# Between the dense steps and the experts: a gather ahead of the first, held weight loads, first rows and activations by halves, fillers at y's copies

## What is computed

```python
x = attention(q, k, v)                    # 2 x 8 heads, 768 positions, 4 sinks, window 128
h = x @ w_in                              # 512 -> 2048, the dense layer
g = np.maximum(h, 0.0) + alpha * np.minimum(h, 0.0)
x = g @ w_out                             # 2048 -> 512: "y" in the kernel
logits = x @ w_gate                       # 8 experts
expert_idx = np.argmax(logits, axis=1)
for i in range(N):                        # in order of tokens
    e = expert_idx[i]
    if counts[e] < capacity:              # 384
        disp[e, counts[e]] = x[i]
        pos[i] = counts[e]; counts[e] += 1; keep[i] = True
h = np.maximum(np.einsum('ecd,edf->ecf', disp, w1), 0.0)
y = np.einsum('ecf,efd->ecd', h, w2)
out[i] = gate_w[i] * y[expert_idx[i], pos[i]]     # rows that were kept
```

## Time and profile before

| | us |
|---|---|
| median of 3 runs | 606.51 |
| lowest, highest | 605.64, 608.17 |
| the profiled execution | 607.66 |
| its span, first to last instruction | 605.9 |
| PE busy in it | 585.7 (97%) |
| mean granted clock of PE | 0.988 of full speed |

### The profile page before, as it was taken

One profiled execution on the slowest core, in us unless ns is written; L12 is line 12 of the kernel. 1 busy time (PEld: TensorE's weight loads), 2 busy tenths in 40 slices (PEclk: granted clock), 3 DMA queues, 4 the chain that ended last, 5 costly groups with the idle time before them and its releaser, 6 DMA issues.

```text
span 605.9 us, 11537 instructions
## 1 busy us (share of the span) xinstructions
PE 585.7 (97%) x3848; PEld 497.4 (82%) x3848; DVE 362.0 (60%) x1063; ACT 276.7 (46%) x681; POOL 147.2 (24%) x244
## 2 busy tenths in 40 slices
PE   8999999999999999999999999998999999989994
PEld 7787878888888888888888899987788888868883
DVE  5878886575556565766565445465826396588200
ACT  5865555342433334333432121142826487697320
POOL 5311332222111221222223100005103243453001
PEclk9999999999999999999999999989999999989998
DMA  7534443001152302010000230027836589597000
GB/s 192 151 94 151 132 126 85 1 18 38 34 158 70 89 18 71 18 36 19 36 18 2 86 123 1 2 87 227 317 136 197 189 294 371 162 393 253 18 21 19
DMA packets 73271, 67.44 MB, mean 111 GB/s; under 512 B 42884, under 2 KB 49044, under 8 KB 73200
## 3 DMA queue, kind: packets, MB, share of 16 engines
q1 hardware_dynamic: 68464, 57.50, 30.0%
q0 software_dynamic: 3680, 8.77, 4.6%
q10 hardware_dynamic: 1056, 0.26, 0.2%
HBM read 57.75 MB, written 12.06 MB: 115 GB/s over the span
## 4 chain that ended last, share of the span: by engine, by line
PE 86%; DVE 6%; issue 3%; ACT 3%; DMA 2%; POOL 0%; SPq 0%; DVEq 0%; POOLq 0%; ACTq 0%
PE bank L1003 22%; PE bank L1005 21%; PE bank L1004 21%; PE bank L993 10%; PE bank L1078 4%; PE bank L1047 4%; PE bank L1146 2%; DVE wl L1355 1%; ACT wh L738 1%; DVE fw L1560 1%; DVE fw L1565 1%; DMA fw<-y_scratch,mask 1%; DVE fw L1398 1%; DMA o_sb<-in_q_dram 1%; DVE rw L1376 1%
## 5 line engine op out<-in xcount | busy, mean ns | idle before, releaser
L1003 PE MATMUL bank<-wh,rw 128*128 128x512 f32 x416 | 167.9, 404 | 3.2 <-DVE rw L1571 1.3
L1005 PE MATMUL bank<-wh,rw 128*128 128x512 f32 x416 | 163.8, 394 | 0.0
L1004 PE MATMUL bank<-wl,rw 128*128 128x512 f32 x416 | 163.6, 393 | 0.0
L1003 PE MATMUL bank<-rw,wh 128*128 128x256 f32 x384 | 112.7, 294 | 0.0
L1005 PE MATMUL bank<-rw,wl 128*128 128x256 f32 x384 | 108.3, 282 | 0.0
L1004 PE MATMUL bank<-rw,wh 128*128 128x256 f32 x384 | 108.0, 281 | 0.0
L879 ACT CAST rw<-fw 128x256 fp32r<-128x256 f32 x96 | 39.0, 406 | 148.2 <-DVE fw L1565 147.9
L1003 PEld LDWEIGHTS bank<-wh,rw 128*128 128x128 f32 x416 | 78.8, 189 | 17.9 <-DVE rw L1571 3.7
L1005 PEld LDWEIGHTS bank<-wh,rw 128*128 128x128 f32 x416 | 78.5, 189 | 17.3
L1004 PEld LDWEIGHTS bank<-wl,rw 128*128 128x128 f32 x416 | 78.7, 189 | 12.6
L1355 DVE TENSOR_TENSOR wl<-fw,wh 128x512 fp32r<-128x512 f32 x127 | 81.4, 687 | 10.0 <-ACT wh L738 7.3
(11 more groups left out here) (124 smaller groups left out, 674.7 us busy)
## 6 DMA issues: line engine op xcount, KB each, us to landing
fw<-in_moe_w_dram SPq DMA_DIRECT2D x95, 256.0 KB, 5.5
v_raw<-in_moe_w_dram SPq DMA_DIRECT2D x22, 256.0 KB, 6.1
fw<-in_moe_w_in_dram SPq DMA_DIRECT2D x16, 256.0 KB, 3.0
fw<-in_moe_w_out_dram SPq DMA_DIRECT2D x16, 256.0 KB, 2.6
y_scratch<-fw SPq DMA_DIRECT2D x12, 256.0 KB, 2.1
out_dram<-v_or_route SPq DMA_DIRECT2D x12, 256.0 KB, 3.5
v_raw<-in_v_dram SPq DMA_DIRECT2D x11, 256.0 KB, 3.0
o_sb<-in_q_dram SPq DMA_DIRECT2D x11, 256.0 KB, 3.3
```

Source lines behind the costliest of these rows:

```text
L1003: pe.matmul(dst, ah, bh, start=start, stop=False, skip_group_check=True)
L1004: pe.matmul(dst, ah, bl, start=False, stop=False, skip_group_check=True)
L1005: return pe.matmul(dst, al, bh, start=False, stop=stop, skip_group_check=True)
```

## The change

Six edits, all at the seam.

1. POOL makes a one-column tile of zeros, `first_row`, at the program's start. Ahead of the first gather it issues an indirect DMA that reads row 0 of `y_scratch` 128 times into the fifth gather buffer, once the first 10 of 12 tiles of y are stored and DVE has copied the last chunk's logits. `gather(4)`, which writes the same buffer, waits for it.
2. SP waits for the first gather to land before it asks for weight piece 14, and so for all after it.
3. The activation of the last dense step is made by halves of 128 columns, one for each token tile, and `y_sum(95, 0)` waits for the first half alone.
4. Three fillers stand ahead of each of the last two `y_T`.
5. The first gathered tile is transposed into two PSUM banks, two 128-column blocks each, and split by halves of 256 columns; `expert_in(0)` waits for each half where it first needs it.
6. `relu(0)` takes its first half when that half's matmuls have ended, and no longer waits for both.

```diff
--- before.py
+++ after.py
@@ -182,2 +182,3 @@
         counts = sb("counts", [P, E], I32)
+        first_row = sb("first_row", [P, 1], U32)
         gid = mask[:, 0, 0:2 * NA].bitcast(U32).rearrange("p (a b) -> p a b", a=2)
@@ -278,2 +279,12 @@
         last_y_evacuated = sem("last_y_evacuated")
...
         last_yT_evacuated = sem("last_yT_evacuated")
@@ -378,2 +389,7 @@
 
+        def half_of(k, half):
+
+            bank = HT_BANK[0] if k == 0 and half else X_BANK[k % 3]
+            return bank[:, half * D // 2:(half + 1) * D // 2]
+
         def yT_bank(t):
@@ -550,2 +566,3 @@
                     load_piece(NP1 + STG2 - 1)
+                    sp.wait_ge(tokens_gathered[0], 16)
                 load_piece(p)
@@ -625,2 +642,3 @@
             assert done[0] == NCONST, done
+            pool.memset(first_row[:, :], 0).then_inc(first_row_made, 1)
 
@@ -663,2 +681,9 @@
             pool.wait_ge(scores_masked, NH)
+            pool.wait_ge(y_stored, 16 * TPC * (NC - 1))
+            pool.wait_ge(first_row_made, 1)
+            pool.wait_ge(router_steps, RS * (NC - 1) + 1)
+            pool.indirect_dma_start(
+                out=x_slot[GR - 1], out_offset=None, in_=y_dram,
+                in_offset=bass.IndirectOffsetOnAxis(ap=first_row[:, 0:1], axis=0),
+                bounds_check=N - 1, oob_is_err=False).then_inc(rows_read_ahead, 16)
             pool.wait_ge(index_steps, 1)
@@ -668,2 +693,4 @@
                 i = X_ORDER[k]
+                if k == GR - 1:
+                    pool.wait_ge(rows_read_ahead, 16)
                 if k >= GR:
@@ -874,3 +901,9 @@
                 m = NF * c + i + 1
-                if 0 <= m < NF * NC:
+                if m == NF * NC - 1:
+                    act.wait_ge(last_half_activated, 1)
+                    act.wait_ge(y_done, m - 1)
+                    act.copy(g_hl[m % 2][:, 0, 0:P], g_full[:, m % 2, 0:P]).then_inc(last_half_high_split, 1)
+                    act.wait_ge(activation_done, m + 1)
+                    act.copy(g_hl[m % 2][:, 0, P:CW], g_full[:, m % 2, P:CW]).then_inc(activation_high_split, 1)
+                elif 0 <= m < NF * NC:
                     act.wait_ge(activation_done, m + 1)
@@ -906,7 +939,15 @@
 
+            def first_x_high():
+                act.wait_ge(first_x_half_transposed, 1)
+                act.copy(eT[0][:, 0, 0:D // 2], half_of(0, 0)).then_inc(first_x_half_high_split, 1)
+                act.wait_ge(slot_x_transposed, 1)
+                act.copy(eT[0][:, 0, D // 2:D], half_of(0, 1)).then_inc(slot_x_high_split, 1)
+
             def relu(i):
-                act.wait_ge(expert_hidden_done, i + 1)
                 if i:
+                    act.wait_ge(expert_hidden_done, i + 1)
                     act.wait_ge(expert_hidden_transposed, 2 * i)
                 for c in range(2):
+                    if i == 0:
+                        act.wait_ge(*((first_hidden_half_done, 1), (expert_hidden_done, 1))[c])
                     act.activation(h_sb[:, c * 512:(c + 1) * 512], H_BANK[c][:, :],
@@ -934,3 +975,3 @@
             busy.load(range(E))
-            x_high(0)
+            first_x_high()
 
@@ -1115,4 +1156,7 @@
                 c, f = divmod(m, NF)
+                if m == NF * NC - 1:
+                    pe.wait_ge(*((last_half_low_split, 1), (activation_low_split, m + 1))[tt])
                 if tt == 0:
-                    pe.wait_ge(activation_low_split, m + 1)
+                    if m < NF * NC - 1:
+                        pe.wait_ge(activation_low_split, m + 1)
                     if c == 0:
@@ -1237,2 +1281,3 @@
             for t in range(NT - TPC, NT):
+                keep_busy(3, H_BANK[0])
                 y_T(t, NH)
@@ -1256,3 +1301,6 @@
                 for kk in range(KC):
-                    r = tr(X_BANK[k % 3][:, kk * P:(kk + 1) * P], x_slot[k % GR][:, kk * P:(kk + 1) * P])
+                    half, at = divmod(kk, KC // 2)
+                    r = tr(half_of(k, half)[:, at * P:(at + 1) * P], x_slot[k % GR][:, kk * P:(kk + 1) * P])
+                    if k == 0 and kk == KC // 2 - 1:
+                        r.then_inc(first_x_half_transposed, 1)
                 r.then_inc(slot_x_transposed, 1)
@@ -1262,4 +1310,4 @@
                 k = X_AT[i]
-                pe.wait_ge(slot_x_low_split, k + 1)
                 if i:
+                    pe.wait_ge(slot_x_low_split, k + 1)
                     pe.wait_ge(expert_relu_done, 2 * i)
@@ -1267,2 +1315,4 @@
                     for kk in range(KC):
+                        if i == 0 and kk % (KC // 2) == 0:
+                            pe.wait_ge(*((first_x_half_low_split, 1), (slot_x_low_split, 1))[kk * 2 // KC])
                         if j == 0:
@@ -1276,2 +1326,4 @@
                     r.then_inc(expert_hidden_done, 1)
+                elif i == 0:
+                    r.then_inc(first_hidden_half_done, 1)
 
@@ -1514,2 +1566,22 @@
 
+            def last_activation(m):
+                hb, g, al = hidden_of(m), g_full[:, m % 2, :], alpha_sb[:, m % NF:m % NF + 1]
+                lo, hi = slice(0, P), slice(P, CW)
+                dve.wait_ge(hidden_done, m + 1)
+                dve.wait_ge(activation_high_split, m - 1)
+                dve.tensor_scalar(g_neg[:, lo], hb[:, lo], 0.0, al, ALU.min, ALU.mult).then_inc(last_half_negative, 1)
+                dve.wait_ge(last_half_negative, 1)
+                dve.scalar_tensor_tensor(out=g[:, lo], in0=hb[:, lo], scalar=0.0, in1=g_neg[:, lo],
+                                         op0=ALU.max, op1=ALU.add).then_inc(last_half_activated, 1)
+                dve.tensor_scalar(g_neg[:, hi], hb[:, hi], 0.0, al, ALU.min, ALU.mult).then_inc(negative_part_done, 1)
+                dve.wait_ge(negative_part_done, m + 1)
+                dve.scalar_tensor_tensor(out=g[:, hi], in0=hb[:, hi], scalar=0.0, in1=g_neg[:, hi],
+                                         op0=ALU.max, op1=ALU.add).then_inc(activation_done, 1)
+                dve.wait_ge(last_half_high_split, 1)
+                dve.tensor_tensor(g_hl[m % 2][:, 1, lo], g[:, lo], f32(g_hl[m % 2][:, 0, lo]),
+                                  ALU.subtract).then_inc(last_half_low_split, 1)
+                dve.wait_ge(activation_high_split, m + 1)
+                dve.tensor_tensor(g_hl[m % 2][:, 1, hi], g[:, hi], f32(g_hl[m % 2][:, 0, hi]),
+                                  ALU.subtract).then_inc(activation_low_split, 1)
+
             def head_step(c, i, n):
@@ -1556,3 +1628,5 @@
                 m = NF * c + i + 1
-                if 0 <= m < NF * NC:
+                if m == NF * NC - 1:
+                    last_activation(m)
+                elif 0 <= m < NF * NC:
                     hb = hidden_of(m)
@@ -1568,3 +1642,3 @@
                     choose(c - 1)
-                if 0 <= m < NF * NC:
+                if 0 <= m < NF * NC - 1:
                     dve.wait_ge(activation_high_split, m + 1)
@@ -1613,2 +1687,10 @@
 
+            def first_x_low():
+                dve.wait_ge(first_x_half_high_split, 1)
+                dve.tensor_tensor(eT[0][:, 1, 0:D // 2], half_of(0, 0), f32(eT[0][:, 0, 0:D // 2]),
+                                  ALU.subtract).then_inc(first_x_half_low_split, 1)
+                dve.wait_ge(slot_x_high_split, 1)
+                dve.tensor_tensor(eT[0][:, 1, D // 2:D], half_of(0, 1), f32(eT[0][:, 0, D // 2:D]),
+                                  ALU.subtract).then_inc(slot_x_low_split, 1)
+
             def hidden_low(i):
@@ -1624,3 +1706,3 @@
             busy.load(range(E // 2))
-            x_low2(0)
+            first_x_low()
 
```

10 lines of the change are left out of this document (added).

## The result

The changed kernel takes 601.1 us (median of 6 runs, 600.59 to 602.12) against 606.83 for the kernel before in the same series (6 runs, 605.64 to 608.17); the ratio is 0.9906, with a 95% interval of 0.989 to 0.9921. That is 5.7 us, where 2.6 were forecast; the time lies just under the forecast range. The profiled execution took 602.12 us with a span of 600.4, 5.5 less than the span of before.

A forecast was written before the change was run, and what follows sets the result against it. PE bounds the kernel nearly everywhere, so time is to be had only at its waits, half clock or fillers at the seam. Terms 0.3 + 1.56 + 0.31 + 0.4 = 2.6 give 606.5 - 2.6 = 603.9 us; 8-in-10 range 601.3 to 606.3.

The forecast's parts named there:

- the sum: Gains at the seam, 0.3 + 1.56 + 0.31 + 0.4 = 2.6 us, expected to be kept to the end.
- Last activation by halves, fillers: Last dense activation and y's last copies: DVE-to-PE path 1.89 to 1.57 us; both edits together give 0.3.
- The first gather: Extra gather ahead and held weights: landing 3.2 us after its start, ending PE's wait of 1.56 us.
- First rows and first relu by halves: First expert's start: 0.31 us of waiting for the gathered tile's split goes, and 0.4 us at the first relu.
- The held pieces: Weight pieces from 14 on, delayed on SP: cost put at nothing, with some 3.5 us of slack left.
- The clock is held: Rival: new fillers prevent the clock's fall at the seam, 2.1 us on top of 2.6, giving 601.8; chance 0.30.
- The gather is still waited for: Rival: first gather lands later than 4.08 us after its start; gain 1.7 or less, 604.8 to 606.5; chance 0.15.

The follow-up runs named there:

- run 8: Kernel before plus eight fillers in a never-taken branch, moving the experts' code 18 instructions further on: 605.43 us, ratio 0.9975.
- run 7: Changed kernel without the six fillers ahead of the counts' loads, experts' code 1 instruction further on than in the kernel before: 604.52 us, ratio 0.9962.
- 3: Changed kernel without SP's wait for the first gather: 601.62 us, ratio 0.9894.
- 4: Changed kernel without the extra gather of row 0 ahead of the first, weights still held: 601.27 us, ratio 0.9913.
- 6: Changed kernel with the six fillers at y's last two copies moved ahead of the counts' loads: 601.48 us, ratio 0.9918.
- 17: Changed kernel with 4 fillers per count in place of 5, and 7 fillers that never run: 600.98 us, ratio 0.991.
- 14: Changed kernel with the last dense activation done whole again: 603.95 us, ratio 0.995.
- 5: Changed kernel without the three fillers ahead of each of the last two transposes of y: 605.21 us, ratio 0.9958.
- 18: Changed kernel with 4 fillers per count in place of 5, and 35 fillers that never run: 599.73 us, ratio 0.9876.
- 10: Kernel before plus 33 fillers in a never-taken branch, moving the experts' code 68 instructions further on: 604.28 us, ratio 0.9953.
- 9: Kernel before plus 27 fillers in a never-taken branch, moving the experts' code 56 instructions further on: 605.1 us, ratio 0.998.
- 11: Changed kernel plus 27 fillers in a never-taken branch, 56 more instructions of code: 601.9 us, ratio 0.9912.
- 15: Changed kernel with the last dense activation done whole again, repeated for a second profile: 602.73 us, ratio 0.9931.
- 16: Changed kernel with the first gathered rows and the first relu done whole again: 603.76 us, ratio 0.9941.

## Why the prediction was wrong

**The step that failed** is the one under the sum: "Behind the seam PE never waits for weights or tiles for long, so I expect it to be kept to the end". It is true of weights and tiles, and PE waited 2.08 us for neither. The sum had no term for the tail, which gave 2.5 of the 5.5 us between the two spans. It rests on a misreading: the prediction says that the earlier trace rows has one slice below 9 in the middle. It has a second, slice 35, and I didn't look into it.

**What stood in its place.** The edits added 13 instructions to PE's stream, and that alone shortens the branch (run 8 adds nothing else; run 7 has all of the edits without the shift, and the long branch). Where the clock doesn't fall behind the wait, the stretch from the 8th to the 11th scaled tile takes 39.7 to 40.0 us at places 0 to 2 and 37.9 to 39.1 at places 11 to 18: 1.4 us less in the mean, not the 2.5 of the two profiles. The fall of the clock behind the wait added 1.6 us in the profiled execution of before (41.5 against 39.9).

Over all runs the clock can only be read as a mean per run. In the five series above it is 0.989 or less in 38 of 108 runs of the kernel before, and in 1 of 33 of the changed kernel, 3, 4, 6 and 17. Among the runs with 0.995 or more (21 and 17) the median spans are 603.8 and 599.5, so about 4.3 us of the gain are there without the falls. That is also the sum of the stretches: 2.3 at the seam, 0.6 at the relu, 1.4 in the tail. The rest of the 5.7, some 1.4, would then be the clock's; that part is read off means and not shown by a run of its own.

**Last activation by halves, fillers: right.** DVE to PE 1.51 for 1.57 (the prediction's own terms add up to 1.61, a slip of the sum); to the logits 0.32 earlier for 0.3, and 0.38 in 14. The fillers at the copies earn nothing that 6 can show.

**The first gather: right in the changed kernel, and too small as a term.** PE's wait went to 0, and the gather landed after 3.6 (forecast 3.2, at most 4.08). But 1.56 was one execution's wait. Six profiles of kernels with this seam unchanged show 1.56, 2.37, 1.49, 2.31, 1.10 and 3.10, a mean of 2.0. Of the two edits only the hold could be seen (0.3 to 0.5 in 3); the gather ahead did what was forecast on POOL, 1.66 to 1.01, and no time hangs on it (4).

Nor do the two edits make the landing certain. In eight profiles that have both it takes 3.6 to 3.8 us; in 5, 6 and 7, which have both too, 5.2, 5.6 and 4.3, and PE waited 0.61, 0.97 and 0.23. In these three a packet of instructions starts while the gather runs (at 413.7, 412.0 and 412.6); in the eight it starts before 409.8, ahead of the gather. So the place of the code, or the time at which PE reaches it, seems to act on the seam as well. That is a coincidence of eleven profiles, and no run separates it.

**First rows and first relu by halves: right in the trace** (0.31 gone; 0.69 and 12 transposes to 0.25 and 8, 0.4 to 0.5). Undoing them cost 2.1 to 2.7, by the late update of PE's semaphore and the clock behind it, which no row of before shows.

**The held pieces** cost nothing, as argued.

**The rivals.** *The clock is held* did not happen and was priced too high: with a fall 17 has a seam of 19.70, without one 18 has 19.02, so the fall costs 0.7 and not 2.1. PE then waits 0.41 and 0.48 between the fillers. In the kernel before even that is free: its seam takes 22.7 and 22.9 us with the fall (before and 10) and 21.9 and 22.7 without it (8 and 9), since PE waits for the gather either way. *The gather is still waited for* did not happen in the changed kernel, but did in 5, 6 and 7, at 0.2 to 1.0 us. Nothing became slower. That the forecast's direction and mechanism at the seam were right does not make the time right.

**What stays open.** Why the semaphore's update behind the first transposes comes 1.5 us late in 11, 14, 15 and 16 and not in the sixteen other profiles; I name no cause. When PE asks for a packet of code, and so why places 11 to 56 are alike and 67 to 69 are not: the trace shows only when the packet starts. Why 7 is 3.4 us slower than the changed kernel by the medians, when in the profiles its seam is 0.6 shorter and its tail 0.7 longer; the 0.9 between the two profiled spans says less than it seems, since that of the changed kernel is the slowest of its 6 runs and that of 7 the third fastest of 12.

## What to carry to other kernels

Read every slice of the page in which PE is under 9, not only the one that the change touches, and ask of each what an edit elsewhere would do to it: a wait with the releaser "issue" beside a branch of microseconds can move with the number of instructions ahead of it; look for a packet on the instruction queue inside the branch. So a comparison of two kernels at 1% needs a control with the same place, such as fillers in a branch that is never taken; without it, six fillers here seemed to be worth 3 to 4 us. And a wait that is to be removed should be read from more than one execution: this one was between 1.1 and 3.1 us.

## What was unexpected of the hardware

- A branch of PE took 0.21 to 0.33 us as a rule (minimum and median of the rows above), 2.5 to 3.5 in four to six places of every trace, and up to 5.5 in one, with the DMA engines full. There it ended 1.34 to 1.47 us after the landing of a 16 KB packet of instructions, in all 20 profiles. 18 instructions that never run made it 4.0, and 68 made it 1.0; with lighter loads at the old place it took 3.1.
- A wait of 2.1 us of PE was followed by a fall of the granted clock to the 1.2 GHz level in one of two profiles of the same kernel, and not behind the waits of 1.8 and 2.1 in 5 and 7.
- The update of PE's semaphore, and with it ACT's first copy of the gathered rows, came 0.3 to 0.4 us after the start of the last transpose that the copy needed (16 profiles) or 1.8 to 1.9 us after it (4), by kernel.
